# A three-part block on one core: x loaded in 512-byte runs, weight slices fetched by GpSimd, and relu-square moved to ScalarE

## The chip, the cores and the metric

One Trainium2 chip, one core. The metric is the device time of one launch in microseconds (us). It is the median of 3 runs. Matrix products run on TensorE (PE), elementwise work on VectorE (DVE), ScalarE (ACT) and GpSimd (POOL). SyncE (SP) issues most DMAs.

## The reference

Three computations follow one another. Only the last is touched by the change.

```
a   = attention(q, k, v) with 4 sink keys and a window of 128     # (3072, 512)
x   = mixture of 8 experts on the rows of a that pass a skip test # (3072, 512)
h   = x @ w_in                 # w_in  (512, 2048)
g   = relu(h) ** 2
out = g @ w_out                # w_out (2048, 512), out (3072, 512)
```

All data are 32-bit floats.

## The kernel before

**The last stage.** Both products of the last part are made by the seven-product scheme for 2 x 2 blocks (Strassen's, in Winograd's form), so each of seven products `p` works on sums of blocks of x and of the weights. Each operand is split into an upper part (`xh`, `w_hi`, rounded) and a lower part (`xl`, `w_lo`, the remainder), and each product is made as three: lower weights by upper data, upper by upper, upper by lower data. One product is 12 matmuls of 128 x 128 by 128 x 512.

**The first layer** (`x @ w_in`) runs in `STEPS` = 12 steps `t`: three thirds `m` of the tokens (1024 each) by four quarters of the columns. TensorE takes the products in the order 1, 5, 6, 2, 7, 4, 3 (in step 0: 1, 2, 5, 6, 7, 4, 3), and `s_one` counts their halves. Results stand in four pairs of PSUM banks, `pa` to `pd`. The other engines turn them into four blocks of g:

- `p1_copy(t)` (ACT, L1086) copies product 1 out of `pa` into `q1`. Product 2 adds to the same banks and waits for this copy.
- `block11(t)` (ACT, L1092 and L1094) makes relu and square of `pa` into `q4`.
- `u2` (DVE, L1919) adds product 6, and product 7 waits for it. `u3_z22` (L1925, L1930) follows product 7, and product 3 waits for it. `z21` (L1941) follows product 4. `z12` (L1947) follows product 3, and product 5 of the next step waits for it.
- After each of `z22`, `z21`, `z12`, `relu_square` (DVE, L1935) turns the block `q3`, `q1`, `q2` into g in place.
- SP stores each block in DRAM (`store_g`, L629), in the order `q4`, `q3`, `q1`, `q2`. `p1_copy` of the next step waits until `q1` has been stored, since it overwrites it.

**The weights.** They are cut into eight column slices: two arrive earlier, and the six others are numbered `k` = 0 to 5. For each, SP loads four blocks into the tile `w_in8` (`load_slice`, L584 and L585), GpSimd makes four sums (`weight_sums`, L864 to L869), ACT rounds to `w_hi` in three pieces (`slice_upper`, L1080), and DVE makes `w_lo` (`slice_lower`, L1912). This happens in steps 1, 2, 9, 10 and 11 for slices 0 to 4, and behind step 11 for slice 5. Slices 0 and 1 complete the first layer's weights. Slices 2 to 5 are the second layer's and take the place of weights that have been used.

**The x blocks.** SP loads x of a third by 32 DMAs of 64 KB (`load_x`, L592), in runs of 32 floats = 128 bytes. DVE turns them by transposes of 32 x 32 (`turn_first` L1893, `turn_later` L1900), and `x_sum` (L1887), `x_upper` (ACT, L1064) and `x_lower` (DVE, L1883) make the operands. Half of x for the first third comes another way, through TensorE transposes; the other half is `first_in`. SP issues the loads for thirds 1 and 2 in steps 2 and 5, ahead of the stores of that step.

**The second layer** (`g @ w_out`) runs in 84 units, four to a product; a unit has 12 matmuls too (L1514, L1515, L1519). `unit_upper` (ACT, L1110) and `unit_lower` (DVE, L1956) make its operands from g read back from DRAM. Its unit 4 needs `w_lo` of slice 5. Output is turned on DVE (L1982) and stored by SP (`store_y`, L668), in runs of 128 bytes.

Each engine runs its program in the written order, and semaphores alone hold them together.

Of the kernel before, what the change touches and what calls it, by code (L numbers as in the profile page):

```python
# [25 lines left out]
P = 128  # L26
# [34 lines left out]
OPENING = (1, 2, 5, 6, 7, 4, 3)  # L61
STEPS, QUARTERS, PIECES = 12, 4, ((1, 3), (3, 5), (5, 8))
# [21 lines left out]
def build(nc, n_sink, window, qT, kT, v, v_sink, w_route, weights, first_w, later_w, out):  # L84
# [11 lines left out]
    with ctx:  # L96
# [106 lines left out]
        early_b12 = at("early_b12", [P, 2, SUPER], F32, blocks_at[SLOTS[7][1]])  # L203
# [72 lines left out]
        s_xin = [sem(f"s_xin{n}") for n in range(4)]  # L276
# [107 lines left out]
        s_closed = {id(e): sem(f"s_closed{n}") for n, e in enumerate((nc.vector, nc.gpsimd, nc.tensor, nc.sync, nc.scalar))}  # L384

# [95 lines left out]
        def _(eng):  # L481
# [100 lines left out]
            def load_slice(k):  # L582

                eng.dma_start(w_in8[:, 0:2, :], later_w[k, :, 0:2, :]).then_inc(s_win, 16)  # L584
                eng.dma_start(w_in8[:, 4:7:2, :], later_w[k, :, 2:4, :]).then_inc(s_win, 16)  # L585

            def load_x(m, n, c, to, done):

                first = m * BOTH + n * SUPER
                rows = x_rows[first:first + SUPER, :].rearrange("(g t) (c b f) -> b t c g f", t=BLOCK, b=P // BLOCK, f=BLOCK)  # L590
                for b in range(P // BLOCK):
                    eng.dma_start(to[b * BLOCK:(b + 1) * BLOCK, :, :], rows[b, :, c, :, :]).then_inc(done, 16)  # L592

# [65 lines left out]
            def store_y(m, which):  # L659

                rows, half_d = {"z11": (0, 0), "z22": (1, 1), "z21": (0, 1), "z12": (1, 0)}[which]
                for half in range(2):
                    n = y_number(m, which, half)
                    eng.wait_ge(s_yturn, n + 1)
                    first, c = m * BOTH + rows * SUPER, 2 * half_d + half
                    to = out[first:first + SUPER, :].rearrange("(g t) (c b f) -> b t c g f", t=BLOCK, b=P // BLOCK, f=BLOCK)
                    for b in range(P // BLOCK):
                        eng.dma_start(to[b, :, c, :, :], y_b[n % 3][b * BLOCK:(b + 1) * BLOCK, :].rearrange("p (g f) -> p g f", f=BLOCK)).then_inc(s_yout[n % 3], 16)  # L668

            load_slice(0)  # L670
# [3 lines left out]
            for c in range(DC):  # L674
                load_x(0, 1, c, first_in[c], s_cx[c])

            x_order = ((0, 0), (0, 1), (1, 0), (1, 1), (0, 2), (0, 3), (1, 2), (1, 3))
            for t in range(STEPS):
                if t in (2, 5):
# [5 lines left out]
                    for n, (token_half, c) in enumerate(x_order):  # L685
# [1482 lines left out]
```

## Time and profile before

| | |
|---|---|
| median of 3 runs | 920.34 us (919.03 to 921.26) |
| the profiled execution | 921.18 us, of which the span is 919.5 us |
| busy in the span | PE 853.1, DVE 680.8, ACT 454.9, POOL 121.5 us |
| granted TensorE clock, mean | 0.972 of full speed |
| first layer and start of the second | 390.2 us to 687.8 us of the span |

A busy PE in the profile is a matmul in flight, at whichever clock was granted. What tells of lost time is the waits, and how many matmuls a stretch holds.

### The profile page before, as it was taken

To read this page: it belongs to the slowest core of one execution; us is meant where nothing else is said; L and a number is where in the kernel's file an instruction comes from. 1 tells how busy PE (TensorE), PEld (TensorE's weight loads), DVE (VectorE), ACT (ScalarE), POOL (GpSimd) and SP (SyncE) were. 2 spreads that over 40 slices of the span, in tenths; PEclk is the share of its full clock that TensorE was granted. 3 is DMA by queue.
4 is the path that set the end of the run, shared out by engine and by line. 5 is a ranking of instruction groups with operands and counts; after the bars stand their busy time and mean duration, and the time that the engine had idled before them with its cause. 6 is when DMAs were issued, how large, how long until landed. Compare 5 with 4: busy or idle time off the path is not lost.

```text
span 919.5 us, 16261 instructions
## 1 busy us (share of the span) xinstructions
PE 853.1 (93%) x4960; PEld 690.0 (75%) x4961; DVE 680.8 (74%) x1533; ACT 454.9 (49%) x900; POOL 121.5 (13%) x170
## 2 busy tenths in 40 slices
PE   9999999999999999969959999977869999999996
PEld 7778777767888887748837878766657888888885
DVE  5787899876777769667748578754479779868964
ACT  7888999855666668332214113222233434334341
POOL 3112222233211123110200000022220000000000
PEclk9999999999999999989979999989979999999999
DMA  5556665187566686332462553322474683576433
GB/s 200 173 165 211 229 224 174 70 287 272 202 225 238 246 289 227 119 68 95 137 158 92 148 151 136 121 108 92 161 274 145 175 224 115 167 198 168 137 78 61
DMA packets 142678, 155.34 MB, mean 169 GB/s; under 512 B 99869, under 2 KB 99997, under 8 KB 142608
## 3 DMA queue, kind: packets, MB, share of 16 engines
q1 hardware_dynamic: 136320, 138.65, 47.7%
q0 software_dynamic: 6000, 15.49, 4.8%
q8 instruction: 36, 0.59, 0.3%
q10 hardware_dynamic: 288, 0.34, 0.1%
q14 instruction: 34, 0.28, 0.1%
HBM read 108.13 MB, written 50.73 MB: 173 GB/s over the span
## 4 chain that ended last, share of the span: by engine, by line
PE 72%; DVE 8%; DMA 5%; issue 4%; SPq 3%; ACT 3%; POOL 2%; DVEq 1%; ACTq 0%; POOLq 0%
PE banks L1519 8%; PE banks L1514 8%; PE banks L1515 8%; PE banks L1344 8%; PE banks L1363 7%; PE banks L1478 5%; PE banks L1479 5%; PE banks L1483 5%; PE banks L1191 4%; PE banks L1246 4%; PE banks L1219 4%; DMA w_in<-in_later_w 3%; SPq L592 3%; DVE w_lo L1912 2%; PE banks L1257 1%
## 5 line engine op out<-in xcount | busy, mean ns | idle before, releaser
L1478 PE MATMUL banks<-xh,w_lo 128*128 128x512 f32 x336 | 137.5, 409 | 39.9 <-DVE q L1930 15.6
L1514 PE MATMUL banks<-xh,w_lo 128*128 128x512 f32 x336 | 132.1, 393 | 5.6 <-ACT xh L1110 5.6
L1479 PE MATMUL banks<-xh,w_hi 128*128 128x512 f32 x336 | 135.6, 404 | 0.0
L1515 PE MATMUL banks<-xh,w_hi 128*128 128x512 f32 x336 | 131.8, 392 | 0.0
L1478 PEld LDWEIGHTS banks<-xh,w_lo 128*128 128x128 f32 x336 | 66.1, 197 | 58.7 <-issue 18.9
L1483 PE MATMUL banks<-xl,w_hi 128*128 128x512 f32 x336 | 107.2, 401 | 0.0
L893 ACT ACTIVATE prob<-score,neg_max 128x264 f32<-128x264 f32 (+1 forms) x192 | 94.0, 496 | 14.0 <-DVE neg_max L1575 13.9
L1519 PE MATMUL banks<-xl,w_hi 128*128 128x512 f32 x336 | 90.0, 390 | 1.1 <-DVE xl L1956 1.1
L1838 DVE TENSOR_TENSOR w_lo<-w_raw,w_hi x70 | 81.9, 1220 | 10.3 <-ACT w_hi L1008 8.2
L1110 ACT ACTIVATE xh<-chain_g 128x1024 fp32r<-128x1024 f32 x48 | 50.8, 1060 | 71.8 <-PE banks L1519 59.6
L1575 DVE CUSTOM_DVE_ANT_0 score<-banks,masks 128x264 f32<-128x264 f32 (+1 forms) x192 | 74.1, 401 | 11.6 <-PE banks L1191 7.8
L1514 PEld LDWEIGHTS banks<-xh,w_lo 128*128 128x128 f32 x336 | 63.9, 190 | 19.3 <-issue 6.0
L1483 PEld LDWEIGHTS banks<-xl,w_hi 128*128 128x128 f32 x336 | 65.7, 196 | 14.7 <-DVE xl L1883 0.5
L1479 PEld LDWEIGHTS banks<-xh,w_hi 128*128 128x128 f32 x336 | 66.3, 197 | 13.7
L1519 PEld LDWEIGHTS banks<-xl,w_hi 128*128 128x128 f32 x336 | 63.1, 188 | 14.8 <-DVE xl L1956 1.7
L1515 PEld LDWEIGHTS banks<-xh,w_hi 128*128 128x128 f32 x336 | 63.8, 190 | 13.3
L1086 ACT ACTIVATE q<-banks 128x1024 f32<-128x1024 f32 x12 | 12.3, 1026 | 122.3 <-DMA g_rows<-q 99.5
L1008 ACT ACTIVATE w_hi<-w_raw x70 | 68.9, 1049 | 3.1 <-issue 3.1
L1956 DVE TENSOR_TENSOR xl<-chain_g,xh 128x1024 fp32r<-128x1024 f32 x48 | 58.3, 1217 | 16.0 <-ACT xh L1110 16.0
L1219 PE MATMUL banks<-ident,prob 128*128 128x128 f32 x352 | 55.3, 280 | 3.7 <-ACT probT L906 3.0
L906 ACT ACTIVATE probT<-banks 128x512 f32<-128x512 f32 (+1 forms) x96 | 53.2, 555 | 6.7 <-PE banks L1219 6.7
L1191 PE MATMUL banks<-k_in,q_in 64*128 64x264 f32 (+1 forms) x384 | 52.8, 391 | 0.3 <-DVE neg_max L1575 0.3
(194 smaller groups left out, 1641.4 us busy)
## 6 DMA issues: line engine op xcount, KB each, us to landing
w_raw<-in_weights SPq DMA_DIRECT2D x64, 512.0 KB, 5.5
g_rows<-q SPq DMA_DIRECT2D x48, 512.0 KB, 2.6
stream_g<-g_rows SPq DMA_DIRECT2D x36, 512.0 KB, 4.0
q_in<-in_qT SPq DMA_DIRECT2D x24, 256.0 KB, 3.1
v_in<-in_v SPq DMA_DIRECT2D x24, 256.0 KB, 3.5
x_rows<-x_row SPq DMA_DIRECT2D x24, 256.0 KB, 3.1
w_in<-in_later_w SPq DMA_DIRECT2D x12, 512.0 KB, 5.7
chain_g<-g_rows SPq DMA_DIRECT2D x12, 512.0 KB, 5.5
```

The source lines that it names most:

```text
L893: eng.activation(prob[:, i % 2, h, 0:width(i)], score[:, i % 2, h, 0:width(i)], ACT.Exp, bias=neg_max[:, i % 2, h:h + 1], scale=-1.0, accu ...
L1191: eng.matmul(score_ps[n % SCORE_BANKS][:, 0:width(i)], q_in[rows, i % 3, h // 2, :], keys, start=True, stop=True).then_inc(s_score, 1)
L1219: ins = eng.transpose(to[:, u * P:(u + 1) * P], prob[:, i % 2, 2 * k + half, at * KB + NS:(at + 1) * KB], ident[:, :])
L1344: ins = eng.matmul(h_ps[half][:, :], x[:, c, :], w[:, c, cols], start=(c == 0 and k == 0), stop=(c == DC - 1 and k == 2))
L1478: eng.matmul(to, w(w_lo, j, c), xh[p][:, c, :], start=(c == 0 and p in (1, 5, 6, 4)), stop=False, skip_group_check=True)
L1479: eng.matmul(to, w(w_hi, j, c), xh[p][:, c, :], start=False, stop=False, skip_group_check=True)
L1483: ins = eng.matmul(to, w(w_hi, j, c), xl[p][:, c, :], start=False, stop=(c == 1), skip_group_check=True)
L1514: eng.matmul(to[c], w(w_lo, j, c), hi[:, j, :], start=(q == 0 and j == 0 and p in (1, 5, 6, 4)), stop=False, skip_group_check=True)
L1515: eng.matmul(to[c], w(w_hi, j, c), hi[:, j, :], start=False, stop=False, skip_group_check=True)
L1519: ins = eng.matmul(to[c], w(w_hi, j, c), lo[:, j, :], start=False, stop=(q == 3 and j == 1), skip_group_check=True)
L1575: eng.tensor_tensor_reduce(score[:, i % 2, h, 0:width(i)], score_ps[n % SCORE_BANKS][:, 0:width(i)], masks[:, mask_kind(i), 0:len(blocks(i ...
L1838: eng.tensor_tensor(w_lo[1 - slot][:, f, :], w_raw[:, f, :], w_hi[1 - slot][:, f, :].bitcast(F32), ALU.subtract).then_inc(s_wlo, 1)
```

## The change

Three edits of the last stage, and one of the end.

1. **x in 512-byte runs.** A third's x is loaded by 8 DMAs of 256 KB in runs of 128 floats. The feature that stands in a partition is another one (a permutation, which the rows of `w_in` follow), so that DVE's transposes and TensorE's 16 first transposes read their input with a step of four floats. The operands are then read and written as runs of 32 floats. `first_in` is loaded by four DMAs, two from SP and two from ACT.
2. **Slices loaded by GpSimd.** `load_slice` leaves SP's program and stands in GpSimd's, ahead of each slice's sums; slice 3 is loaded into the unused part of the raw weights' memory (`IN_PLACE`), and slice 4 is loaded ahead of it.
3. **relu and square on ScalarE.** For `q3`, `q1`, `q2` DVE's one pass becomes two ACT passes, Relu and Square. In steps 1, 2, 9 and 11 `slice_upper` moves ahead of `p1_copy`, and `slice_lower` ahead of `u2`; in step 10 they stand behind `block11` and `z21`.
4. **The last store** is split: two DMAs of each half from SP, two from ACT.

```diff
-                eng.wait_ge(s_win, 32 * k + 32)
-            for k in range(6):
-                weight_sums(k)
+            load_slice(0)
+            weight_sums(0)
+            eng.wait_ge(s_wpl, 3)
+            load_slice(1)
+            weight_sums(1)
+            eng.wait_ge(s_xl, x_made(2, 3))
+            load_slice(2)
+            weight_sums(2)
+            eng.wait_ge(s_wpl, 9)
+            load_slice(4)
+            weight_sums(4)
+            eng.wait_ge(s_one, halves(9, 3))
+            load_slice(3)
+            weight_sums(3)
+            eng.wait_ge(s_wpl, 15)
+            load_slice(5)
+            weight_sums(5)
...
+            def relu_square(t, q, source, ready, made, stored):
+                eng.wait_ge(*ready)
+                if stored is not None:
+                    wait(eng, stored, 16 * t)
+                eng.activation(q[:, :, :], source, ACT.Relu).then_inc(made, 1)
+                eng.wait_ge(made, 2 * t + 1)
+                eng.activation(q[:, :, :], q[:, :, :], ACT.Square).then_inc(made, 1)
...
+        def load_x(eng, m, half, b, to, done):
+            first = m * BOTH + half * SUPER
+            rows = x_rows[first:first + SUPER, b * P:(b + 1) * P].rearrange("(g t) f -> t g f", t=BLOCK)
+            eng.dma_start(to[b * BLOCK:(b + 1) * BLOCK, :, :], rows).then_inc(done, 16)
...
-                eng.transpose(x_turned[n // 2][:, n % 2, :], x_in[n][:, :, :].rearrange("p g f -> p (g f)")).then_inc(s_xturn, 1)
+                part = slice(n * DC, n * DC + DC)
+                eng.transpose(x_turned[half][:, part, :].rearrange("p g (c t) -> p g c t", t=BLOCK),
+                              x_in[half][:, part, :].rearrange("p g (f c) -> p g c f", f=BLOCK)).then_inc(s_xturn, 1)
```

ACT's program from step 10's copy of product 1 to step 11's. `q_78` to `q_81` are `q1` to `q4`. Before:

```order
L1086 ACTIVATE q_78<-banks 128x1024 [waits s_st21,s_one]
L1080 ACTIVATE w_hi<-w_in_101 128x2x512 [waits s_wsum,s_one] x2
L1080 ACTIVATE w_hi<-w_in_101 128x3x512 [waits s_wsum,s_one]
L1092 ACTIVATE q_81<-banks 128x1024 [waits s_st11,s_one]
L1094 ACTIVATE q_81<-q_81 128x1024 [waits s_g11]
L1086 ACTIVATE q_78<-banks 128x1024 [waits s_st21,s_one]
```

And now, where L1129 is that copy, L1136 and L1138 are Relu and Square and L1123 is `slice_upper`:

```order
L1129 ACTIVATE q_78<-banks 128x1024 [waits s_st21,s_one]
L1136 ACTIVATE q_81<-banks 128x1024 [waits s_st11,s_one]
L1138 ACTIVATE q_81<-q_81 128x1024 [waits s_g11]
L1123 ACTIVATE w_hi<-raw_lo 128x2x512 [waits s_wsum,s_one] x2
L1123 ACTIVATE w_hi<-raw_lo 128x3x512 [waits s_wsum,s_one]
L1136 ACTIVATE q_80<-q_80 128x1024 [waits s_z22]
L1138 ACTIVATE q_80<-q_80 128x1024 [waits s_g22]
L1136 ACTIVATE q_78<-q_78 128x1024 [waits s_z21]
L1138 ACTIVATE q_78<-q_78 128x1024 [waits s_g21]
L1136 ACTIVATE q_79<-q_79 128x1024 [waits s_z12]
L1138 ACTIVATE q_79<-q_79 128x1024 [waits s_g12]
L1123 ACTIVATE w_hi<-w_in_90 128x2x512 [waits s_wsum,s_one] x2
```

Behind that row stand the third piece of slice 4 and step 11's copy. Six passes and slice 4's three pieces have come between the two copies, and slice 3 has moved behind `block11`.

GpSimd's program of the slices 2 and 4 now (slice 3 follows). Before, it held only the four TENSOR_TENSOR of each slice, the first waiting for `s_win`:

```order
L889 DMA w_in_90<-in_later_w 128x1024 [waits s_xl]
L889 DMA w_in_90<-in_later_w 128x2x512
L895 TENSOR_TENSOR w_in_90<-w_in_90 128x512 [waits s_win]
L896 TENSOR_TENSOR w_in_90<-w_in_90 128x512
L898 TENSOR_TENSOR w_in_90<-w_in_90 128x512 [waits s_wsum]
L900 TENSOR_TENSOR w_in_90<-w_in_90 128x512 [waits s_wsum]
L889 DMA w_in_90<-in_later_w 128x1024 [waits s_wpl]
```

Each load now stands behind the sums of the slice before it, and waits for its own condition and no longer for SP's stores.

DVE's program from `z22`'s second half to the end of step 10 now (L1999, L2005 and L2011 are `z22`, `z21` and `z12`, L1981 is `slice_lower`):

```order
L1999 TENSOR_TENSOR q_80<-q_78,banks 128x512 [waits s_u3]
L2005 TENSOR_TENSOR q_78<-q_78,banks 128x1024 [waits s_z22,s_one]
L1981 TENSOR_TENSOR w_lo<-raw_lo,w_hi 128x2x512 [waits s_wph] x2
L1981 TENSOR_TENSOR w_lo<-raw_lo,w_hi 128x3x512 [waits s_wph]
L2011 TENSOR_TENSOR q_79<-q_79,banks 128x1024 [waits s_u2,s_one]
```

Here the three squaring passes are gone, and slice 3's lower parts, which stood ahead of `u3_z22`, stand ahead of `z12`.

## Rows read from the trace of the kernel before

**Rows 1.** Waits of PE, 350 to 700 us: total us, times, longest

```profile
PE banks L1478 <- DVE q L1930: 15.6, 3, 5.3
PE banks L1478 <- ACT q L1086: 11.8, 2, 10.6
PE banks L1478 <- ACT xh L1064: 6.1, 2, 5.5
PE banks L1514 <- ACT xh L1110: 5.6, 1, 5.6
PE banks L1478 <- DVE q L1947: 5.0, 4, 1.7
...
PE banks L1478 <- DVE q L1919: 1.4, 1, 1.4
PE banks L1519 <- DVE xl L1956: 1.1, 1, 1.1
```

**Rows 2.** Timeline of PE: start, us, operation, idle time before it

```profile
390.19 0.50 PE L1478 MATMUL banks<-xh,w_lo 128*128 128x512 f32 x1 [0.66 <-ACT xh L1064]
...
429.09 0.39 PE L1478 MATMUL banks<-xh,w_lo 128*128 128x512 f32 x1
...
431.81 0.39 PE L1478 MATMUL banks<-xh,w_lo 128*128 128x512 f32 x1
...
687.81 0.76 PE L1514 MATMUL banks<-xh,w_lo 128*128 128x512 f32 x1 [5.56 <-ACT xh L1110]
```

**Rows 3.** Windows: length, busy of PE, PEld, DVE, ACT, POOL, granted clock, DMA

```profile
390.00:421.00 31.00, 22.67 (x85) 17.25 (x86) 22.62 (x23) 9.35 (x10) 4.83 (x4) 0.89 0.30 68
...
459.00:492.00 33.00, 21.69 (x86) 17.25 (x85) 20.65 (x24) 7.96 (x8) 0.00 (x0) 0.84 0.54 137
492.00:592.00 100.00, 95.70 (x420) 78.33 (x420) 73.85 (x76) 24.22 (x24) 0.00 (x0) 1.00 0.40 128
592.00:674.00 82.00, 66.44 (x256) 53.27 (x255) 43.03 (x42) 21.01 (x20) 15.18 (x12) 0.88 0.39 139
674.00:696.00 22.00, 15.37 (x59) 11.99 (x58) 15.37 (x14) 9.25 (x9) 5.17 (x4) 0.84 0.71 265
```

**Rows 4.** Timelines of SP, ACT and DVE around x's loads

```profile
453.52 18.56 SPq L592 DMA_DIRECT2D x_in<-x_rows  x32
...
477.72 1.02 ACT L1086 ACTIVATE q<-banks 128x1024 f32<-128x1024 f32 x1 [24.55 <-DMA g_rows<-q]
...
532.11 3.16 DVE L1900 STREAM_TRANSPOSE x_turned<-x_in 128x512 f32<-128x512 f32 x4
```

**Rows 5.** Timelines of SP, POOL, ACT and DVE: slice 3 in step 10

```profile
622.25 1.22 SPq L584 DMA_DIRECT2D w_in<-in_later_w  x1
...
628.99 1.28 POOL L864 TENSOR_TENSOR w_in<-w_in 128x512 f32<-128x512 f32 x1 [22.25 <-DMA w_in<-in_later_w]
...
634.22 3.38 ACT L1080 ACTIVATE w_hi<-w_in 128x1024 fp32r<-128x1024 f32 x3 [10.83 <-POOL w_in L869]
...
635.31 4.08 DVE L1912 TENSOR_TENSOR w_lo<-w_in,w_hi 128x1024 fp32r<-128x1024 f32 x3 [6.29 <-ACT w_hi L1080]
```

**Rows 6.** Timelines of SP, DVE and ACT: `first_in`

```profile
390.28 8.30 SPq L592 DMA_DIRECT2D first_in<-x_rows  x16
...
400.30 0.71 DVE L1893 STREAM_TRANSPOSE early_b<-first_in 128x512 f32<-128x512 f32 x1 [1.22 <-DMA first_in<-x_rows]
...
402.15 1.06 ACT L1064 ACTIVATE xh<-early_chain 128x1024 fp32r<-128x1024 f32 x1 [2.22 <-DVE early_chain L1887]
```

**Rows 7.** Groups by line, 390 to 690 us: busy us, mean ns, idle before

```profile
L1935 DVE SCALAR_TENSOR_TENSOR q<-q 128x1024 f32<-128x1024 f32 x36 | 44.5, 1236 | 1.2
...
L1094 ACT ACTIVATE q<-q 128x1024 f32<-128x1024 f32 x12 | 12.7, 1060 | 0.4
```

**Rows 8.** DMA issues: KB each, us from issue to landing

```profile
g_rows<-q SPq DMA_DIRECT2D x48, 512.0 KB, 2.6
...
x_res<-routed POOLq DMA_DIRECT2D x15, 260.0 KB, 6.3
```

**Rows 9.** Timeline of SP at the end: the last stores

```profile
897.67 19.93 SPq L668 DMA_DIRECT2D out<-y_b  x17
```

More of the change, by code:

```diff
@@ L384, in build, with store_y @@
         s_closed = {id(e): sem(f"s_closed{n}") for n, e in enumerate((nc.vector, nc.gpsimd, nc.tensor, nc.sync, nc.scalar))}
+        def store_y(eng, m, which, blocks_of):
+            rows, half_d = {"z11": (0, 0), "z22": (1, 1), "z21": (0, 1), "z12": (1, 0)}[which]
+            for half in range(2):
+                n = y_number(m, which, half)
+                eng.wait_ge(s_yturn, n + 1)
+                first, c = m * BOTH + rows * SUPER, 2 * half_d + half
+                to = out[first:first + SUPER, :].rearrange("(g t) (c b f) -> b t c g f", t=BLOCK, b=P // BLOCK, f=BLOCK)
+                for b in blocks_of:
+                    eng.dma_start(to[b, :, c, :, :], y_b[n % 3][b * BLOCK:(b + 1) * BLOCK, :].rearrange("p (g f) -> p g f", f=BLOCK)).then_inc(s_yout[n % 3], 16)
+        def load_x(eng, m, half, b, to, done):
+            first = m * BOTH + half * SUPER
+            rows = x_rows[first:first + SUPER, b * P:(b + 1) * P].rearrange("(g t) f -> t g f", t=BLOCK)
+            eng.dma_start(to[b * BLOCK:(b + 1) * BLOCK, :, :], rows).then_inc(done, 16)
         def close(eng):
@@ L657, in load_stream @@
                 load_g(m, blk, q, stream_g[q], s_stream[q // 2])
[L659 to L670, printed above, removed]
             eng.wait_ge(s_bscatter, tiles * 16 + 16)
@@ L729, in _ @@
                 if m >= 1:
-                    store_y(m - 1, "z12")
+                    store_y(eng, m - 1, "z12", range(4))
                 for q in range(QUARTERS):
@@ L739, in _ @@
                         load_b12(m + 1, q)
-                store_y(m, "z22")
+                store_y(eng, m, "z22", range(4))
                 if m < 2:
@@ L1114, in _ @@
             eng.wait_ge(s_cturn, 2)
-            x_upper(0, 1, x_source(0, 1))
+            x_upper(0, 1)
             eng.wait_ge(s_cturn, 4)
-            x_upper(0, 2, x_source(0, 2))
+            x_upper(0, 2)
             eng.wait_ge(s_bscatter, tiles * 16 + 16)
             close(eng)
+            for b in range(2, 4):
+                load_x(eng, 0, 1, b, first_in, s_xin[2])
             for t in range(STEPS):
+                if t in (1, 2, 9, 11):
+                    for piece in range(3):
+                        slice_upper({1: 0, 2: 1, 9: 2, 11: 4}[t], piece)
                 p1_copy(t)
@@ L1169, in _ @@
                             product_one(m)
+            store_y(eng, 2, "z12", (2, 3))
         @block.tensor
@@ L2054, in _ @@
+                    x_sum(b11_x, b12_x, b11_x)
                 if t in (4, 8):
-                    x_lower(m, 2, xt[2])
-                    x_lower(m, 7, xt[1])
-                u2(t)
-                if t in (1, 2, 9, 10, 11):
+                    x_lower(m, 2)
+                    x_lower(m, 7)
+                if t in (1, 2, 9, 11):
+                    for piece in range(3):
+                        slice_lower({1: 0, 2: 1, 9: 2, 11: 4}[t], piece)
+                u2(t)
+                if t in (3, 7):
+                    x_lower(m + 1, 5)
+                    x_sum(b11_x, b22_x, b11_x)
+                    x_sum(b12_x, b22_x, b12_x)
```

248 lines of the change are left out of this document (129 added, 119 removed).

## The prediction

> **What bounds the kernel now.** I read the windows first, then the waits of PE, then the timelines of the engines named there. TensorE is the bound: where nothing holds it up, one product starts 2.72 us after the one before [rows 2], so a step of seven products is 19.04 us. Between the first product at 390.19 us and the fourth unit of the second layer at 687.81 us [rows 2] lie 297.6 us, and in them 84 products and 3 units, which is 87 x 2.72 = 236.6 us of work. So 61.0 us are lost there. PE's waits in the same stretch [rows 1] sum to 46.6 us; without the 0.66 ahead of the first product and the 1.1 behind the fourth unit's start, 44.9. The other 16.1 us are matmuls at the lower of the clock's two levels behind the long waits. The windows show it: the granted clock is 0.89, 0.84, 0.88 and 0.84 in the four stretches that hold a wait of over 5 us, and 1.00 from 492 to 592 us, where the waits are short [rows 3]. A wait of 1.7 us costs itself, and one of 5 us costs about half as much again. Two things have to be kept apart: which waits go, and whether what is left of one stays short.
>
> **Where each wait comes from.** Three waits of 5.2 us, for `z22` (L1930), in steps 9 to 11: DVE stands in `slice_lower`, which waits for ACT, which waits for GpSimd's sums, which wait for SP's load. From the load's issue to ACT's first piece are 634.22 - 622.25 = 12.0 us, and `slice_lower` adds 4.1 [rows 5]. SP issues the load behind the last store of the step before, so it comes too late in each step. A fourth, 5.6 us ahead of unit 4, is the same with slice 5. One of 10.6 us is in step 3: SP spends 18.56 us on 32 DMAs of x, the stores of step 2 stand behind them in its queue, and the copy of product 1 waits for the store of `q1` [rows 1, 4]. One of 5.5 us is in step 0: 16 DMAs take SP 8.3 us, and product 5 waits for transposes, sum and rounding [rows 1, 6]. The short ones for `z12` (5.0 us in 4) come from transposes ahead of it on DVE, and from `relu_square` passes.
>
> **x in longer runs.** 8 DMAs instead of 32. No row has 512-byte runs. With 64 KB in 512 runs a DMA took SP 18.56 / 32 = 0.58 us [rows 4], and the new ones have 512 runs of 256 KB each. If issuing is paid by the run, a third's x takes 8 x 0.58 = 4.6 us; if it is paid by the byte, at the old rate, 18.6 us. I take 5, since the stores move 512 KB in 2.6 us [rows 8] and so bytes are not the limit of the DMA engines. The load also starts earlier, since `slice_lower` of slice 1 ends about 9 us into step 2. It is over about 14 us into the step, when the first store of the step is just ready. The 10.6 us wait goes. The cover is thin only if the byte price holds: then SP is free at +28, and the wait returns with some 5 us.
>
> **Step 0.** SP issues its two at about 390.3 us, ACT its two at 391.1. GpSimd's load of slice 0 (1 MB), which was done by now, starts at 388.7 and shares the engines: both megabytes should be in by 396, bounds 394.5 and 398. Then two transposes (1.4), a sum (1.2) and the rounding (1.1) give product 5 at 400 instead of 403.3, and the wait is 2 us instead of 5.5. After it product 6 waits about 2.3 and product 7 about 1.9, because transposes and sums follow one another on DVE (before, the slow clock covered them). I get step 1 at 418.0 instead of 420.9: step 0 loses 8.8 us over its 19.04.
>
> **relu and square.** DVE loses 3 x 1.24 = 3.7 us a step, ACT gains 3 x 2 x 1.06 = 6.4 us and then holds 9.5 of 19.04 [rows 7]. Only its order matters. With +0 the start of a step: the pass pair for `q3` starts at z22 of the step before; that for `q1` ends so that the store (2.6 us, [rows 8]) lands at about +4.2; `z12` runs +0.2 to +1.4, and the pair for `q2` ends at +3.6. The copy of product 1 may then run at +4.3, and product 2 needs it at +8.16. That is 2.8 us of slack in a plain step, after the copy itself. Where `slice_upper` (3.4 us) stands ahead of the copy, it ends at +7.0 and the copy at +8.1: no slack. In steps 1 and 2 the sums are ready in time (slice 1: `w_lo` of slice 0 at about +8.7, then 12 us). I charge 0.1. DVE without its squares frees `z12`; four transposes (3.2 us, [rows 4]) still stand ahead of it in steps 2 and 5 and leave 0.2 each. With 0.5 for the steps 3, 4, 7 and 8, where x's parts are made, steps 1 to 8 lose 1.0 us. If the runs of 32 floats or the step of four floats slow DVE, this grows (a rival below).
>
> **Slices 2, 4, 3.** GpSimd's load of slice 2 waits for the last `x_lower` of step 8: `u2` ends at about +10.2 (the store of `q2` lands at +8.9), two `x_lower` at +12.5. Twelve microseconds on, ACT begins at 24.5, which is +5.5 of step 9. GpSimd's own DMAs are seen at 6.3 us for 260 KB beside other loads [rows 8], so I leave the 12 us with 11.6 to 15 as its bounds. `slice_upper` ends at +8.9, the copy at +9.9: product 2 waits 1.8 us (1.4 to 4.8). `slice_lower` is done at +10.7, slice 4 is summed at step 10's +1.5, and slice 3 is fetched next and ready at about +14. ACT does it until +17.3, `z22` having come at +16.2, and DVE makes its lower parts from +17.6 to +21.7. `z12` runs behind them to +22.9, while product 5 of step 11 wants it at 21.76: 1.2 us. ACT's pair for `q2` ends at 25.1, slice 4 at 28.4, the copy at 29.5, and product 2, by then due at 28.4, waits 1.1. Slices 3 and 4 so cost 2.3 us. Slice 5 is issued at +11.3 of step 11; 12.5 us later are +23.8; its first piece, the pair for `q2`, two more pieces and `unit_upper` take 6.7, and unit 4 is due at about +29.5: 1.0 (0 to 3).
>
> **The sum.** The stretch becomes 236.6 + 8.8 + 1.0 + 1.8 + 2.3 + 1.0 = 251.5 us against 297.6: 46.1 less. Behind unit 4 the 1.1 us wait for `xl` and about 2 us of slow matmuls [rows 1, 3] have gone with the long wait; I take 2.5. At the end SP alone issues 17 DMAs in 19.9 us, the last eight back to back [rows 9]; two queues start the last four pairs together, and at 0.58 us each [rows 4] the bounds are 0 and 4 x 0.58 = 2.3; I take 1.3. In all 49.9: 921.2 - 49.9 = 871.3 for the profiled execution, whose 921.18 stands 0.8 above the median of 920.34. I say 871.
>
> The Trainium skill speaks against the third edit: ScalarE: Activation LUTs, Rules for kernel authors, wants relu and multiplications on VectorE, not ScalarE. By this trace too it is the dearer place (2.12 us against 1.24), but DVE's time is on TensorE's path there and ACT's is not. By that rule moving the passes back would be the faster kernel, by at most what ACT's order now costs, the 0.1, 1.8 and 1.1 us above.
>
> **Rivals.**
>
> *Strided reads slow* (12%). The transposes and TensorE's first loads of x read with a step of four floats. No row shows such a read. If each took twice as long, the four transposes ahead of `z12` in steps 2 and 5 would add 3.2 us each, those in steps 3 and 6 push `u2` late by up to 3, step 0 gains 2, and the start of the stage up to 2: about 14 us, 885. For it speaks only that nothing bounds it from above; against it, that elements and not bytes set the time of DVE's other forms (1.24 us for 1024 whether one input or two). The Trainium skill, SBUF — State Buffer, Door 1: The DMA port swizzle, says that accesses that cross to a new 16-byte line pay a penalty. A step of four floats does this at each element, so by that page this rival is the case; no run yet shows it.
>
> *The slices stay late* (15%). GpSimd loads and sums in series, three slices from +12.5 of step 8 to +14 of step 10. If a load by GpSimd takes 3 us more than SP's, the waits in step 9 (4.8) and 11 (about 4) and ahead of unit 4 (4) are long enough for the low clock: 8 us of waits more and 4 of clock, 883.
>
> *ScalarE becomes the bound* (3%), slower than before. The copy of product 1 stands behind six passes. It costs once the copy is ready over 2.8 us later than I have it; to lose all of the gain each of 11 steps must be late by 2.8 + 49.9 / 11 = 7.3 us. Only a pass of Relu or Square that took twice its 1.06 us (6.4 us a step more, four of them ahead of the copy) comes near. Then 925. Against it: Square on this very shape runs at 1.06 today [rows 7], and Relu in the same pair.
>
> *Nothing changes* (1%): the waits are not what SP's order and the slices make of them. [Rows 5] speak against it.
>
> **How the numbers follow.** My forecast has 69%. Its own bounds are -3 (no wait in step 9, slice 5 hidden, tail 2.3) and +8. The two rivals at 883 and 885 are in the range: 864 to 889. Outside are the slower case and the tails. A difference of 0.2% (1.8 us) is about what a measurement tells from no change: faster 0.96, same 0.01, slower 0.03.
>
> **What would show it.** Waits of PE: L1930's three, and the 10.6 us for the copy in step 3, are gone; what is left are waits for the copy in steps 9 and 11 of 1 to 2 us, one for `z12` in step 11 and three of about 2 in step 0. SP issues x in some 5 us. The granted clock is 1.00 from step 1 to 11. Transposes stay at 0.71 us, ACT's passes at 1.06. I am wrong if the transposes are longer, if a GpSimd load and sums take over 13 us, or if a wait of 5 us remains.

## The result and the profile after

| | before | after |
|---|---|---|
| median | 920.44 us (919.03 to 921.26, 4 runs) | 886.37 us (883.84 to 888.17, 4 runs) |
| profiled execution, its span | 921.18, 919.5 us | 883.84, 882.4 us |
| busy: PE, DVE, ACT, POOL | 853.1, 680.8, 454.9, 121.5 us | 841.7, 648.2, 529.1, 127.5 us |

The ratio is 0.9629 (0.9599 to 0.966): 34 us less. The direction and the range held; the forecast of 871 was 15 us too low.

The waits of PE in the changed kernel, from 370 to 700 us: engine, tile and line waited for, total us, times, longest. They answer to [rows 1].

```profile
PE banks L1543 <- ACT xh L1112: 7.8, 3, 6.3
PE banks L1543 <- DVE q L2011: 4.2, 3, 1.7
PE banks L1543 <- ACT q L1129: 3.8, 3, 2.0
PE banks L1543 <- DVE q L1988: 2.6, 2, 1.4
PE banks L1584 <- DVE xl L2020: 2.6, 1, 2.6
PE banks L1579 <- DVE w_lo L1981: 1.4, 1, 1.4
```

L1988 is `u2` (L1919 before), L2011 is `z12` (L1947 before), L1129 the copy, L1112 `x_upper`; `z22`, L1930 before and L1999 now, is no longer among them. The three waits of 5.2 us for it are gone and so is the 10.6 us wait for the copy. One wait over 5 us is left, in step 0. PE's timeline in the stretch:

```profile
388.21 0.50 PE L1543 MATMUL banks<-xh,w_lo 128*128 128x512 f32 x1 [0.64 <-ACT xh L1112]
392.81 0.47 PE L1543 MATMUL banks<-xh,w_lo 128*128 128x512 f32 x1 [1.21 <-ACT q L1129]
402.08 0.80 PE L1543 MATMUL banks<-xh,w_lo 128*128 128x512 f32 x1 [6.29 <-ACT xh L1112]
...
412.47 0.47 PE L1543 MATMUL banks<-xh,w_lo 128*128 128x512 f32 x1 [1.41 <-DVE q L1988]
...
463.42 0.47 PE L1543 MATMUL banks<-xh,w_lo 128*128 128x512 f32 x1 [1.71 <-DVE q L2011]
...
649.91 0.47 PE L1579 MATMUL banks<-xh,w_lo 128*128 128x512 f32 x1 [1.38 <-DVE w_lo L1981]
657.29 1.20 PE L1584 MATMUL banks<-xl,w_hi 128*128 128x512 f32 x4 [2.58 <-DVE xl L2020]
```

From the first product to the fourth unit are now 649.91 - 388.21 = 261.7 us, against 297.6 before [rows 2] and 251.5 in the prediction. The windows (length, busy of PE, PEld, DVE, ACT, POOL, granted clock, DMA share, GB/s) answer to [rows 3]:

```profile
388.00:421.00 33.00, 22.91 (x86) 16.95 (x87) 21.88 (x22) 12.87 (x14) 5.03 (x4) 0.90 0.29 85
...
460.00:480.00 20.00, 18.30 (x81) 14.75 (x80) 19.38 (x20) 10.68 (x11) 0.00 (x0) 1.00 0.28 114
...
630.00:650.00 20.00, 18.62 (x83) 15.12 (x82) 15.10 (x15) 15.77 (x16) 7.22 (x6) 1.00 0.87 314
650.00:660.00 10.00, 7.42 (x29) 5.74 (x30) 9.75 (x9) 4.69 (x5) 0.00 (x0) 0.93 0.64 238
660.00:875.00 215.00, 214.99 (x945) 177.62 (x943) 171.43 (x157) 82.60 (x78) 0.00 (x0) 1.00 0.52 145
```

The clock is 1.00 from step 1 to unit 4, as forecast (a window from 421 to 649 us has 1.00): what is lost there is waits and the restarts behind them, not the clock. It is below 1.00 only behind the two longest waits.

The transposes of x and the order of DVE's work tell where much of the rest of the forecast went. The transposes as a group of the changed kernel, 388 to 650 us (x, busy us, mean ns, idle before); [rows 4] had 4 of this shape in 3.16 us:

```profile
L1967 DVE STREAM_TRANSPOSE x_turned<-x_in 128x512 f32<-128x512 f32 x16 | 17.6, 1101 | 1.3
L1959 DVE STREAM_TRANSPOSE early_b<-first_in 128x512 f32<-128x512 f32 x4 | 4.1, 1073 | 7.1 <-DMA first_in<-x_rows 7.1
```

And the timeline of DVE in step 0, at the turn from step 2 to step 3, in step 10 and around unit 4:

```profile
397.63 2.06 DVE L1959 STREAM_TRANSPOSE early_b<-first_in 128x512 f32<-128x512 f32 x2 [7.08 <-DMA first_in<-x_rows]
399.72 1.22 DVE L1952 TENSOR_TENSOR early_chain<-early_b,banks 128x1024 f32<-128x1024 f32 x1
...
457.45 4.72 DVE L1967 STREAM_TRANSPOSE x_turned<-x_in 128x512 f32<-128x512 f32 x4
462.09 1.18 DVE L2011 TENSOR_TENSOR q<-q,banks 128x1024 f32<-128x1024 f32 x1
...
609.38 1.22 DVE L1988 TENSOR_TENSOR q<-q,banks 128x1024 f32<-128x1024 f32 x1 [9.57 <-DMA g_rows<-q]
...
638.82 4.36 DVE L2020 TENSOR_TENSOR xl<-chain_g,xh 128x1024 fp32r<-128x1024 f32 x2
...
652.61 3.49 DVE L2024 TENSOR_TENSOR chain_g<-b_g,chain_g 128x1024 f32<-128x1024 f32 x3
656.02 1.22 DVE L2020 TENSOR_TENSOR xl<-chain_g,xh 128x1024 fp32r<-128x1024 f32 x1
```

Four transposes of 1.1 us stand ahead of `z12` (L2011), and PE waits for it until 463.42. SP's queue shows the part that went as meant:

```profile
389.18 0.86 SPq L438 DMA_DIRECT2D first_in<-x_rows  x2
...
448.49 5.36 SPq L438 DMA_DIRECT2D x_in<-x_rows  x8
```

A third's x takes SP 5.36 us where it took 18.56 [rows 4].

### The profile page after: what moved, and what is told of

Same layout as the page of the kernel before. It is cut to its first block, busy times and chain, and to the rows that moved or that the text cites. A ratio compares the mean times of both kernels' runs of the same rounds, so it can differ in the third digit from the quotient of the medians.

```text
span 882.4 us, 16237 instructions
## 1 busy us (share of the span) xinstructions
PE 841.7 (95%) x4960; PEld 682.2 (77%) x4961; DVE 648.2 (73%) x1497; ACT 529.1 (60%) x972; POOL 127.5 (14%) x184
## 4 chain that ended last, share of the span: by engine, by line
PE 81%; DVE 7%; DMA 5%; issue 3%; ACT 3%; DVEq 0%; ACTq 0%; POOLq 0%; SPq 0%
PE banks L1584 8%; PE banks L1580 8%; PE banks L1579 8%; PE banks L1409 8%; PE banks L1428 7%; PE banks L1543 7%; PE banks L1544 7%; PE banks L1548 7%; PE banks L1256 5%; PE banks L1311 5%; PE banks L1284 4%; PE banks L1322 1%; PE banks L1417 1%; ACT prob L939 1%; PE banks L1336 1%
## 5 line engine op out<-in xcount | busy, mean ns | idle before, releaser
L1543 PE MATMUL banks<-xh,w_lo 128*128 128x512 f32 x336 | 132.9, 396 | 18.5 <-ACT xh L1112 7.8
L1579 PE MATMUL banks<-xh,w_lo 128*128 128x512 f32 x336 | 131.6, 392 | 1.4 <-DVE w_lo L1981 1.4
L1580 PE MATMUL banks<-xh,w_hi 128*128 128x512 f32 x336 | 131.7, 392 | 0.0
L1544 PE MATMUL banks<-xh,w_hi 128*128 128x512 f32 x336 | 131.6, 392 | 0.0
L1548 PE MATMUL banks<-xl,w_hi 128*128 128x512 f32 x336 | 104.2, 391 | 0.1
L1584 PE MATMUL banks<-xl,w_hi 128*128 128x512 f32 x336 | 90.1, 390 | 2.6 <-DVE xl L2020 2.6
L1543 PEld LDWEIGHTS banks<-xh,w_lo 128*128 128x128 f32 x336 | 63.6, 189 | 36.0 <-ACT xh L1112 10.7
L1584 PEld LDWEIGHTS banks<-xl,w_hi 128*128 128x128 f32 x336 | 63.3, 189 | 16.2 <-DVE xl L2020 3.0
L1579 PEld LDWEIGHTS banks<-xh,w_lo 128*128 128x128 f32 x336 | 63.5, 189 | 15.0 <-DVE w_lo L1981 1.8
L1548 PEld LDWEIGHTS banks<-xl,w_hi 128*128 128x128 f32 x336 | 63.2, 189 | 14.4 <-DVE xl L1948 1.0
L1580 PEld LDWEIGHTS banks<-xh,w_hi 128*128 128x128 f32 x336 | 63.5, 189 | 13.2
L1544 PEld LDWEIGHTS banks<-xh,w_hi 128*128 128x128 f32 x336 | 63.7, 189 | 12.9
L2020 DVE TENSOR_TENSOR xl<-chain_g,xh 128x1024 fp32r<-128x1024 f32 x48 | 60.3, 1259 | 16.0 <-ACT xh L1166 16.0
L1136 ACT ACTIVATE q<-q 128x1024 f32<-128x1024 f32 x36 | 38.1, 1058 | 41.2 <-DVE q L1999 28.1
```

Source lines behind the costliest of these rows:

```text
L1543: eng.matmul(to, w(w_lo, j, c), xh[p][:, c, :], start=(c == 0 and p in (1, 5, 6, 4)), stop=False, skip_group_check=True)
L1544: eng.matmul(to, w(w_hi, j, c), xh[p][:, c, :], start=False, stop=False, skip_group_check=True)
L1548: ins = eng.matmul(to, w(w_hi, j, c), xl[p][:, c, :], start=False, stop=(c == 1), skip_group_check=True)
L1579: eng.matmul(to[c], w(w_lo, j, c), hi[:, j, :], start=(q == 0 and j == 0 and p in (1, 5, 6, 4)), stop=False, skip_group_check=True)
L1580: eng.matmul(to[c], w(w_hi, j, c), hi[:, j, :], start=False, stop=False, skip_group_check=True)
L1584: ins = eng.matmul(to[c], w(w_hi, j, c), lo[:, j, :], start=False, stop=(q == 3 and j == 1), skip_group_check=True)
```

## The experiments

Theory A is the prediction's sum, with what the changed kernel showed: each edit takes away the waits named for it, and the strided transposes, the late `first_in` and the late pieces near unit 4 cost the missing time. The rivals are named in each expectation. The twelve kernels ran in three groups of four, each beside the kernel before, which took 921.6 us (first group), 922.2 (second) and 920.9 (third). The table gives the medians and the ratio to it; a difference within a group is surer than one across groups, and the changed kernel's 886.4 us is of a run of its own.

| kernel | median us | ratio, 95% |
|---|---|---|
| only_loads | 900.57 | 0.9711 to 0.9809 |
| only_squares | 922.82 | 0.9997 to 1.0048 |
| only_x | 914.66 | 0.9895 to 0.9942 |
| no_x | 898.60 | 0.9707 to 0.9825 |
| contig_time | 880.14 | 0.9494 to 0.9569 |
| late0 | 889.03 | 0.9591 to 0.9669 |
| dve_order | 881.91 | 0.9516 to 0.9589 |
| best | 882.70 | 0.9539 to 0.9608 |
| no_loads | 914.99 | 0.9919 to 0.9962 |
| no_squares | 899.02 | 0.9748 to 0.9788 |
| sp0 | 883.13 | 0.9567 to 0.9605 |
| sp0_order | 880.53 | 0.9535 to 0.9599 |

### Each edit alone

**only_loads**: the kernel before, with the slices loaded by GpSimd in rising order, all into `w_in8`, at their old places on ACT and DVE.

```
# GpSimd's program; SP's five load_slice calls are gone
+            for k in range(6):
+                if k == 2:
+                    eng.wait_ge(s_xl, x_made(2, 3))
+                elif k > 0:
+                    eng.wait_ge(s_wpl, 3 * k)
+                load_slice(k)
+                weight_sums(k)
```

> The kernel before with one edit: GpSimd loads each weight slice itself, in the order 0 to 5, all into the same tile; x's loads, the squares and the places of the slice work stay. Theory A (the waits are separate, each goes with its own cause): in steps 9 to 11 the slice is summed before ACT wants it, the three waits of 5.2 us for the third product and their slow matmuls go (3 x 8.1 us), the wait ahead of the second layer's fourth unit stays at about 4 us, step 0 loses 1 to 3 us to the shared load: 896 us, 893 to 900. Theory B (the edits need each other: without the squares off VectorE nothing is early enough): less than 5 us gained, 915 or more.

It gained 21 us. The long waits of PE, 370 to 700 us:

```profile
PE banks L1470 <- ACT q L1078: 10.6, 2, 9.4
PE banks L1470 <- ACT xh L1056: 8.7, 2, 8.0
PE banks L1506 <- ACT xh L1102: 7.0, 2, 6.5
```

The three waits for `z22` are gone, as the theory has it. The wait behind SP's x stays (9.4), the one ahead of unit 4 too (6.5, slice 5), and the one in step 0 grew to 8.0 us.

**only_squares**: the kernel before, with the three blocks' relu and square as two passes of ACT (`block22`, `block21`, `block12`) and none on DVE.

```
-                relu_square(q3, (s_z22, 2 * t + 2), s_g22)      # DVE, three blocks
+                block22(t)                                      # ACT: Relu, then Square
```

> The kernel before with one edit: relu and square of the three blocks as two ScalarE passes each; loads and the places of the slice work stay. Theory A: the three slice waits stay, and the loads of slices 3 and 4 start 0.9 us later, since SP issues them behind the store of a block whose passes end later; the short waits behind the squares shrink by 2 to 3 us: 920 us, 917 to 923. Theory B: the squares are what held the last part, and 5 us or more are gained: below 915.

There is no gain. The four waits for `z12` shrank from 5.0 us to one of 1.5, but the three for `z22` came to 18.7 us instead of 15.6, and unit 4's to 8.4 instead of 5.6. In steps 9 to 11 the passes on ACT are not the cause: it sits idle for 11 us until GpSimd's sums are there (timeline of ACT):

```profile
633.93 3.38 ACT L1080 ACTIVATE w_hi<-w_in 128x1024 fp32r<-128x1024 f32 x3 [11.12 <-POOL w_in L869]
```

The slices' loads still stand behind SP's stores, and step 10's restart behind `z22` is 27.4 us behind step 9's in both kernels (641.23 - 613.85 before, 640.95 - 613.56 here). Ahead of unit 4 the pair for `q2` does stand between slice 5's first and second piece on ACT (683.24 and 686.23).

**only_x**: the changed kernel with the loads on SP, the slices at their old places and in their old order, and the squares on DVE.

> The kernel before with one edit: x in 512-byte runs with everything that follows from it (transposes that read with a step of four floats), first_in from two queues, the last store from two queues; slices loaded by SP, squares on VectorE. Theory A: the 10.6 us wait in step 3 and its 2 us of slow matmuls go, step 0 gains 2 to 3, the transposes of 1.1 us instead of 0.71 cost 1.6 us each in steps 2 and 5: 909 us, 906 to 913. Rival: the 10.6 us wait belongs to the store of the first product's block and comes back in another place: 915 or more.

It took 914.7 us, a gain of seven: above theory A's 906 to 913 and near the rival's number, but not by the rival's cause: the wait for the copy is gone, and what came in step 3 is a wait for DVE (timeline of PE):

```profile
466.34 0.77 PE L1527 MATMUL banks<-xh,w_lo 128*128 128x512 f32 x1 [4.44 <-DVE q L2000]
```

and this is what DVE does ahead of it:

```profile
458.31 1.22 DVE L1988 SCALAR_TENSOR_TENSOR q<-q 128x1024 f32<-128x1024 f32 x1
460.46 4.63 DVE L1951 STREAM_TRANSPOSE x_turned<-x_in 128x512 f32<-128x512 f32 x4 [0.92 <-DMA x_in<-x_rows]
465.02 1.18 DVE L2000 TENSOR_TENSOR q<-q,banks 128x1024 f32<-128x1024 f32 x1
```

DVE holds both its squares and the longer transposes ahead of `z12`, and the matmul behind the wait takes 0.77 us: it runs at the lower level.

### Each edit taken back

**no_x**: only_loads and only_squares together.

> The kernel before with the loads by GpSimd (order 0 to 5, one tile) and the squares on ScalarE, without the x edit; the slice work at its old places. Theory A: the gain of the loads alone and 2 to 4 us from the short waits: 893 us, 889 to 897; step 3 keeps its wait of 10 us. Theory B: well over the sum of the two single edits.

It took 898.6 us, above A's 889 to 897. The gain of 23.0 us is 3.3 over the sum of the two single edits, less than only_loads is known to, so it is no clear case of B either. Against only_loads it is 2.0 us less. The waits for `z12` fell from 4.3 us to 1.1, but the one ahead of unit 4 grew from 6.5 to 9.4, and the longest in step 3 stayed at 9.4.

**no_loads**: the changed kernel with SP's `load_slice` calls and the rising order back.

> The changed kernel with the weight slices loaded by SP at the places of the kernel before (all into one tile, order 0 to 5), everything else as changed. Theory A (the slice work ahead of the copy of product 1 is safe only because the slice has been fetched a step ahead): slices 2 and 4 are summed 16 us into steps 9 and 11, the copy stands behind them and product 2 waits about 12 us in each, and ahead of the fourth unit of the second layer again: 916 us (910 to 925). Theory B (the waits of the kernel before come back, no more): 906 or less.

It waits for the copy (L1119) 28.6 us in 5, the longest 13.2: the copy stands behind `slice_upper` on ACT and now waits for SP's slices. So this variant pays for late slices more than the kernel before did.

**no_squares**: the changed kernel with the three squares back on DVE, one pass each.

> The changed kernel with relu and square of the three blocks back on VectorE (one pass each, ahead of the next sum), the slice work at the changed kernel's places. Alone on the kernel before, moving them to ScalarE gained nothing. Theory A (they are worth something only once slices and transposes stand on VectorE's path ahead of the last block's sum): the waits for that sum grow to 4.4 and 3 us in steps 3 and 6 and 3.4 in step 11, one of them with slow matmuls; ScalarE's waits of 2.6 us go: 895 us (891 to 899). Rival: the place of the squares is neutral here too: 884 to 889.

```profile
PE banks L1540 <- DVE q L2013: 11.3, 5, 3.2
PE banks L1540 <- ACT xh L1112: 6.4, 2, 5.8
```

In these waits of PE `z12` costs 11.3 us in 5, against 4.2 in 3 in the changed kernel. The longest are 3.2 and 3.1 us in steps 3 and 6, behind the transposes, and 2.5 in step 11, behind slice 3's lower parts.

The three edits are worth, alone and taken back from the changed kernel (its 886.4 less the variant):

| edit | alone | in the changed kernel |
|---|---|---|
| x in longer runs | 6.9 | 12.2 |
| slices by GpSimd | 21.0 | 28.6 |
| squares on ACT | -1.3 | 12.7 |

Alone they sum to 26.6 us and together they give 34.1. Both figures of the x row hold the split of the last store too, and its 12.2 the placing of the slices, which no_x has as before; the 28.6 holds the cost of late slices ahead of the copy. The 7.5 us between the sums are not well known (the interval of only_loads alone is 4.5 us either way). What is clear of the spread is the squares' change from -1.3 to 12.7 us. That the late slices are gone is not enough for it: between only_loads and no_x the same edit gave 2.0 us. By the rows it takes what the changed kernel has put ahead of `z12` on DVE, the longer transposes and slice 3's lower parts: without the edit `z12` costs TensorE 11.3 us there, and 4.3 in only_loads. No run has one of the two without the other.

### The cost of the strided reads

**contig_time**: DVE's transposes read 128 adjacent floats of a row instead of every fourth. The amount of work and all transfers are unchanged, but the features then meet the wrong rows of the weights: the kernel is for its time only.

```
-                return first_in[:, :, c:P:DC]
+                return first_in[:, :, c * BLOCK:(c + 1) * BLOCK]
-   ... rearrange("p g (f c) -> p g c f", f=BLOCK)
+   ... rearrange("p g (c f) -> p g c f", f=BLOCK)
```

> The changed kernel, with VectorE's transposes of x reading runs of 32 floats instead of single floats four apart. The features are then paired with the wrong rows of the weights, so it is for its time only. Theory A (the step of four floats is what makes a transpose of 128 x 512 take 1.10 us instead of 0.71, and DVE pays this on TensorE's path): transposes at 0.71 us; the two waits of 1.7 us for the last block in steps 3 and 6 fall below 0.3, and step 0 loses 1.4 us less: 4.5 us less than the changed kernel, 882 us (879 to 885). Rival: the longer transposes come from the DMAs that write the same memory meanwhile, or they are hidden: transposes stay above 1.0 us, or the time within 1 us of 886.

```profile
L1967 DVE STREAM_TRANSPOSE x_turned<-x_in 128x512 f32<-128x512 f32 x16 | 11.3, 708 | 1.3
L1959 DVE STREAM_TRANSPOSE early_b<-first_in 128x512 f32<-128x512 f32 x4 | 2.6, 688 | 6.5 <-DMA first_in<-x_rows 6.5
```

A transpose takes 0.71 us again, the waits for `z12` fall from 4.2 us in 3 to 0.9 in 1, and the time by 6.2 us (880.1 against 886.4; by the ratios, which the higher time of the kernel before in this group widens, by 1.0%). The same element count, type and form at a step of four floats takes 1.10 us. So the rival of strided reads was half true: the instruction slows by 0.39 us, not by 0.71, and it costs 6 us, not 14. The Trainium skill, SBUF — State Buffer, Door 1: The DMA port swizzle, says that each access crossing into another 16-byte line pays a penalty. The trace agrees in the direction, with 1.10 against 0.71 us; no run has another step, so that the line of 16 bytes is what sets it is not shown. The rival's other half, TensorE's first reads of x, is there and costs next to nothing: the weight loads that read x with this step take 0.209 us each instead of 0.140, and the 16 transposes over them 0.283 instead of 0.273.

### Step 0

**late0**: GpSimd loads slice 0 only once `first_in` has landed.

```
+            eng.wait_ge(s_xin[2], 16 * (P // BLOCK))
             load_slice(0)
             weight_sums(0)
```

> The changed kernel, with one wait more: GpSimd issues the load of slice 0 only once first_in has landed. Theory A (in step 0 the 1 MB of slice 0 and the 1 MB of first_in share the DMA engines, and product 5 waits for it): first_in lands 2 us sooner, the wait ahead of product 5 falls from 6.3 to about 4.5 us, slice 0 is still summed 10 us ahead of its use: 2 to 3 us less, 884 us. Rival: first_in is slow by its 512-byte runs alone: the wait stays above 6 us, no change.

The wait of product 5 fell from 6.29 to 3.53 us, and yet the kernel was no faster. The timelines of DVE and POOL tell why:

```profile
400.19 1.22 DVE L1949 TENSOR_TENSOR xl<-early_chain,xh 128x1024 fp32r<-128x1024 f32 x1 [1.12 <-ACT xh L1113]
...
405.34 2.29 DVE L1953 TENSOR_TENSOR early_b<-early_b,early_b 128x1024 f32<-128x1024 f32 x1
407.56 2.29 DVE L1949 TENSOR_TENSOR xl<-early_chain,xh 128x1024 fp32r<-128x1024 f32 x1
```

```profile
403.05 1.28 POOL L895 TENSOR_TENSOR w_in<-w_in 128x512 f32<-128x512 f32 x1 [5.75 <-DMA w_in<-in_later_w]
404.30 2.24 POOL L896 TENSOR_TENSOR w_in<-w_in 128x512 f32<-128x512 f32 x1
```

Where GpSimd's sums lie beside DVE's operations on two SBUF tiles, DVE's takes 2.29 us instead of 1.22, and GpSimd's 2.24 instead of 1.28: each lasts nearly as long as both together. TensorE's next wait grew from 0.84 to 1.75 us and a new one of 1.65 us followed, with matmuls at the lower level behind it. From the first product to the restart ahead of product 7 (`u2`) late0 takes 26.0 us (415.09 - 389.11), the changed kernel 24.3 (412.47 - 388.21). The Trainium skill, SBUF — State Buffer, SBUF: two separate sides, describes the port pair that the two engines share as an exclusive lock, not a split; two engines that take turns would show just these lengths, though the records show only the lengths and not the turns.

**sp0**: SP loads slice 0 as in the kernel before, ahead of its wait for the last rows of x from the experts.

```
# SP, ahead of eng.wait_ge(s_bscatter, tiles * 16 + 16)
+            eng.dma_start(w_in8[:, 0:2, :], later_w[0, :, 0:2, :]).then_inc(s_win0, 16)
+            eng.dma_start(w_in8[:, 4:7:2, :], later_w[0, :, 2:4, :]).then_inc(s_win0, 16)
```

> The changed kernel with slice 0 loaded by SP 7 us earlier and nothing else. Theory A: 883 us (881 to 885), 3 us less than the changed kernel's 886. Rival: no change, 885 to 888.

The wait is 3.17 us, no sum of DVE or GpSimd in step 0 is stretched, the same piece of step 0 takes 21.1 us (410.39 - 389.26), and the kernel is 3.2 us faster than the changed one. Both runs take the slice out of `first_in`'s way and both shorten the wait by about 3 us; only the one that does not put GpSimd's sums beside DVE's keeps the gain.

### DVE's order, and the two together

**dve_order**: two of the four transposes go behind `z12` in steps 2 and 5, and unit 5's first lower parts ahead of the sums `t1`.

```
-                    for n in range(4):
+                    for n in range(2):
                         turn_later((t + 1) // 3, 0, n)
...
                 z12(t)
+                if t in (2, 5):
+                    for n in range(2, 4):
+                        turn_later((t + 1) // 3, 0, n)
# ahead of the second layer's loop
+            unit_lower(0, 5, 0)
```

> The changed kernel, with two moves in VectorE's program and no other edit: in steps 2 and 5 only two of the four transposes stand ahead of the last block's sum, two behind it; and behind the last slice the lower parts of the second layer's fifth and sixth units stand ahead of two and one of the three sums that they don't need. Theory A (what is left of TensorE's waits is VectorE's order): the waits in steps 3 and 6 (1.7 and 1.6 us) and the one for the fifth unit's lower part (2.6 us, with slow matmuls behind it) go: 6 us less, 880 us (878 to 883). Rival: the work is only shifted, and u2 or the next slice's lower part is late instead: less than 2 us gained.

The `z12` waits of steps 3 and 6 are gone, a `u2` wait of 1.7 us took the place of one, the wait for `xl` in unit 4 is 0.9 instead of 2.6, and the kernel is 4.5 us faster.

**best**: dve_order and late0.

> The changed kernel with the late slice 0 and VectorE's new order together. If both stand on separate waits, their gains add: 878 us (875 to 881). If step 0's gain is taken back by product 6, whose operand stands behind two more transposes, 880 or more.

No better than dve_order alone: the stretched sums of late0 are there again (2.29 us). **sp0_order** takes sp0 in late0's place:

> The changed kernel with VectorE's new order (as in dve_order), and slice 0 loaded by SP 7 us earlier, as in the kernel before, GpSimd making its sums as soon as it is there. Theory A (two things stood against step 0: the DMA engines shared with slice 0, and, once that load was moved behind first_in, GpSimd's sums beside VectorE's two-input passes in SBUF, both at half speed): no tensor_tensor of step 0 above 1.3 us, the wait ahead of product 5 about 3.5 us, none over 1.5 behind it: 3 us less than dve_order, 879 us (876 to 881). Rival: slice 0's place doesn't matter: within 1 us of dve_order's 882.

With 880.5 us (0.9535 to 0.9599) it beats both kernels, by 40 us the one before and by 6 the changed one. Against dve_order (another group, 881.9) the difference is inside the spread of its six runs, 876.2 to 887.1. Its longest waits of PE are 3.7 us in step 0 and 2.1 for the copy.

## Why the prediction was right, and where it was 15 us off

**Right.** The direction, and which waits go: the three for `z22`, the 10.6 us one, and unit 4's 5.6. SP issues x in 5.36 us (I took 5). ACT's passes take 1.06 us. The clock is 1.00 in steps 1 to 11. A slice by GpSimd takes 12.9 us from issue to ACT (570.14 to 583.03, below) where I had 12, and the wait in step 9 is 2.0 instead of 1.8. ScalarE did not become the bound: the waits for the copy are 3.8 us in 3.

Of the prediction's own three signs of being wrong, two have come: the transposes are longer (1.10 us, not 0.71), and a wait of over 5 us remains (6.29, in step 0). The third, a GpSimd load and sums of over 13 us, came in slice 3 alone, with 13.9 (599.44 to 613.35); slice 2 took 12.8 and the others less. Nor does the measured 886 us speak for the two rivals whose times, 883 and 885, lie nearer to it than 871: the slices are not late, and the strided reads cost 6 us and not 14. It is the sum's own terms that were too small.

The timeline of POOL in the changed kernel, slices 2, 3 and 5:

```profile
570.14 1.27 POOL L889 DMA_DIRECT2D w_in<-in_later_w  x2 [129.62 <-DVE xl L1948]
577.78 1.29 POOL L895 TENSOR_TENSOR w_in<-w_in 128x512 f32<-128x512 f32 x1 [6.38 <-DMA w_in<-in_later_w]
...
599.44 0.55 POOL L883 DMA_DIRECT2D raw_hi<-in_later_w  x1
...
639.94 2.16 POOL L900 TENSOR_TENSOR w_in<-w_in 128x512 f32<-128x512 f32 x1
```

and of ACT:

```profile
583.03 3.38 ACT L1123 ACTIVATE w_hi<-w_in 128x1024 fp32r<-128x1024 f32 x3 [2.40 <-POOL w_in L900]
```

**Off.** The profiled execution is 921.18 - 883.84 = 37.3 us faster, and the sum had 49.9. The stretch has 10.2 us more than forecast, what is behind it 4.6 more, and the first product came 2.0 earlier (388.2; in the kernels with the changed x this start lay between 388.2 and 390.5, and in those with the old one between 388.3 and 392.1, so it is spread and no gain of the change). That is 12.8 of the 12.6 missing, the rest being what lies outside the span. The median is another 2.5 above the profiled run. The terms:

| term | predicted | measured |
|---|---|---|
| step 0 | 8.8 | 13.4 |
| steps 1 to 8 | 1.0 | 3.3 (1.71 and 1.60 for `z12`) |
| step 9 | 1.8 | 2.0 |
| slices 3 and 4 | 2.3 | 2.8 (1.23, 0.94, 0.60) |
| ahead of unit 4 | 1.0 | 1.4 |
| restarts | none | 2.2 |
| behind unit 4, and the tail | -3.8 | +0.8 |

*Step 0* is the largest error of the stretch: 412.47 + 3 x 2.72 = 420.6 is the start of step 1, and 420.6 - 388.2 - 19.04 = 13.4. I had both megabytes in by 396, at most 398; `first_in` is there at 397.6, 8.4 us behind its issue, with slice 0's megabyte ahead of it in the DMA engines, and two transposes take 2.06 us instead of 1.4. The wait was then long enough (6.29) that the matmuls behind it ran at the lower level. late0 and sp0 show that the slice is the larger part of the excess over the 2 us I had: without it beside `first_in` the wait is 3.5 and 3.2. What remains of it has the strided transposes (contig_time: 5.0 with the slice still there).

*Steps 1 to 8*: the mechanism stood in the prediction, with 0.71 us a transpose. At 1.10 four take 4.7 us and `z12` is 1.6 to 1.7 us late, not 0.2. contig_time takes both waits away. The prediction's argument against slow reads, 1.24 us for 1024 elements "whether one input or two", did not bear on them: the pass with one tile's name (L1935) reads that tile as both of its inputs, and no form of those rows reads with a step.

*Restarts*: I charged a wait its own length. Its length is counted from the end of the last matmul, which lies about 0.17 us behind the moment when the next could have started (0.39 us long, one every 0.227), and the product behind it comes slowly into step, 0.34 us from the first matmul to the second and then one each 0.23 (timeline of PE):

```profile
622.81 0.50 PE L1543 MATMUL banks<-xh,w_lo 128*128 128x512 f32 x1 [0.94 <-DVE q L2011]
623.15 0.40 PE L1544 MATMUL banks<-xh,w_hi 128*128 128x512 f32 x1
```

Seven short waits at 0.3 are 2.1 of the 2.2 us. By the same estimate the 12 waits of the kernel before hold 3.6 of the 16.1 us that the prediction put down to the lower level of the clock alone.

*Behind unit 4*: I had the 1.1 us wait for `xl` gone with the long wait ahead of it. It grew to 2.6, with slow matmuls behind it. DVE makes three sums `t1` of unit 4 (3.49 us) ahead of unit 5's lower part, and its work before it was late, since GpSimd's sums of slice 5 lay beside it: at 638.82 two lower parts take 4.36 us, and L900 on POOL 2.16 us instead of 1.29.

dve_order shows the first of these, with 0.9 us left of 2.6. That the stretch of 4.36 us has a share in it is argued from the rows; no run took it away alone.

*The tail*: stores on two queues end the span 4.8 us behind DVE's last turn, where one queue took 5.4. That is 0.6 us of the 1.3 that the prediction took.

*The squares.* The Trainium skill's rule, ScalarE: Activation LUTs, Rules for kernel authors, wants relu and multiplication on VectorE. In this trace the ScalarE form is dearer (2 x 1.06 against 1.24 us), and moving it there alone gained nothing (only_squares, 1.0022). In the changed kernel it is worth 12.7 us (no_squares), since the DVE time stands ahead of `z12`. The prediction had the direction but no price for it: it put the gain of DVE's time into "frees `z12`". The 12.7 us are no share of the 34, since the three edits taken back one by one sum to 53.5. By the rule it named, moving the passes back would have been faster, by at most 3.0 us (0.1, 1.8 and 1.1); the run that does it is slower.

**Open**: whether a store of step 10 that landed about 7 us behind its issue (`q2`; the median of these stores is 2.6) was held by GpSimd's four DMAs of slice 3, which is what the order of events suggests (GpSimd issues from 599.44 to 601.6, SP the store at 602.02, and DVE, which waits for it, starts at 609.38). It made the 1.23 us wait; no run moved it.

## What to carry to other kernels

Ask of every load that is moved to another queue what else it will share the DMA engines and the other engines with at its new time: here slice 0's load and sums cost step 0 some 3 us wherever they met `x` or DVE's sums, and less when it was issued early. Price a change of layout at its reader too, not only at the DMA: 13 us of SP's time were bought with 0.39 us more a transpose, on an engine that had no slack ahead of `z12`. And test an edit that frees an engine together with the others: the same edit gave nothing alone, 2.0 us beside one other edit, and was worth 12.7 us where the others had put more work ahead of `z12` on that engine.

## What the runs showed of the hardware

- STREAM_TRANSPOSE of 128x512 fp32 on VectorE: 0.71 us from adjacent floats, 1.10 us at a step of four floats.
- An fp32 operation of VectorE on two SBUF tiles (128x1024) takes 1.22 us alone and 2.29 beside GpSimd's sums, which go from 1.28 to 2.24 us (128x512).
- What clock follows a wait was not told by its length alone. Behind 2.13 us in sp0_order the matmuls ran at the lower level at once, and behind 3.14 us in no_squares at the upper one. Behind 3.15 us in best the first took 0.50 us and the level fell 0.6 us later (0.62 us a matmul at 401.30).

```profile
583.98 0.78 PE L1548 MATMUL banks<-xh,w_lo 128*128 128x512 f32 x1 [2.13 <-ACT q L1134]
```

```profile
529.46 0.50 PE L1540 MATMUL banks<-xh,w_lo 128*128 128x512 f32 x1 [3.14 <-DVE q L2013]
```

- A third's x (2 MB) in 8 DMAs of 512-byte runs is issued in 5.4 us, and its transfer fills the DMA engines: the windows around it in the changed kernel and in the one before (columns as above) have 201 GB/s at a DMA share of 1.06 against 106 at 0.67.

```profile
448.50:459.00 10.50, 10.50 (x48) 8.71 (x47) 6.25 (x8) 5.52 (x6) 0.00 (x0) 1.00 1.06 201
```

```profile
453.50:472.00 18.50, 14.08 (x62) 11.03 (x60) 12.57 (x15) 0.00 (x0) 0.00 (x0) 1.00 0.67 106
```
